# Turned rows of the hidden layer moved from an SBUF tile into PSUM, one step later, with quarter rows in two buffers

## The reference

```python
logits = x @ w_gate
e_idx = np.argmax(logits, axis=1)
...
for e in range(E):
    mask = e_idx == e
    h = np.maximum(x[mask] @ w1[e], 0.0)
    ye = h @ w2[e]
    out[mask] = gate_w[mask, None] * eom[mask, e, None] * ye
```

## Time and profile before

| what | value |
|---|---|
| median of 3 runs (lowest to highest) | 772.63 us (772.59 to 777.18) |
| the profiled execution's own time | 767.37 us |
| span of the profiled execution, first to last instruction | 765.7 us |
| TensorE busy | 719.5 us, 94% |
| VectorE busy | 492.6 us, 64% |
| ScalarE busy | 306.8 us, 40% |
| granted TensorE clock, mean | 0.99 of full speed |

### The profile page before, as it was taken

The page is one execution under the profiler, slowest core; times in us unless marked ns, Lnnn a source line. Parts: engine busy times, 40 slices in busy tenths (PEclk is TensorE's granted clock), DMA queues, the critical chain, the costliest instruction groups (busy, mean ns, idle before and its releaser), DMA issues.

```text
span 765.7 us, 16189 instructions
## 1 busy us (share of the span) xinstructions
PE 719.5 (94%) x5272; PEld 617.3 (81%) x5273; DVE 492.6 (64%) x777; ACT 306.8 (40%) x467; POOL 188.6 (25%) x352
## 2 busy tenths in 40 slices
PE   3899999999999999999988979999898989999995
PEld 3689998999899899989887767788686868788873
DVE  5787877787767676768716746536757575665441
ACT  3644443444344434443334434134444535363220
POOL 3211543345111211211211212122131312222111
PEclk9999999999999999999999999999999999999998
DMA  8723235323322231231017648442848485843230
GB/s 323 247 70 99 97 112 158 117 96 114 120 69 69 91 115 69 69 107 46 22 38 246 217 131 220 146 110 60 272 110 277 118 251 144 255 90 79 71 72 36
DMA packets 43949, 98.70 MB, mean 129 GB/s; under 512 B 6286, under 2 KB 19982, under 8 KB 43792
## 3 DMA queue, kind: packets, MB, share of 16 engines
q1 hardware_dynamic: 22128, 64.82, 26.2%
q10 hardware_dynamic: 15840, 16.52, 9.4%
q0 software_dynamic: 5952, 16.98, 7.5%
HBM read 73.78 MB, written 14.09 MB: 115 GB/s over the span
## 4 chain that ended last, share of the span: by engine, by line
PE 78%; DMA 7%; DVE 5%; issue 5%; ACTq 2%; DVEq 1%; ACT 1%; POOLq 0%; SPq 0%; POOL 0%
PE banks L1216 65%; DMA r_quads<-r_sb 5%; PE banks L1247 4%; PE banks L1237 3%; PE banks L1269 3%; PE banks L1229 2%; ACTq L724 2%; DVE slots_hi_lo L1162 1%; PE banks L1349 1%; DMA q_sb<-q_t 1%; ACT r_sb L717 1%; DVEq L406 1%; DMA xs<-x_rows,rows_now 1%; DVE xsT_lo L1044 0%; DVE ys_even L1170 0%
## 5 line engine op out<-in xcount | busy, mean ns | idle before, releaser
L1216 PE MATMUL banks<-slots_hi_lo,rT_hi 128*128 128x512 f32 x464 | 146.2, 396 | 2.9 <-DVE rT_lo L1055 2.2
L1216 PE MATMUL banks<-slots_hi_lo,xsT_hi 128*128 128x512 f32 x464 | 128.4, 399 | 15.5 <-DVE xsT_lo L1044 10.4
L1216 PEld LDWEIGHTS banks<-slots_hi_lo,xsT_hi 128*128 128x128 f32 x464 | 86.9, 191 | 39.3 <-issue 21.7
L1216 PEld LDWEIGHTS banks<-slots_hi_lo,rT_hi 128*128 128x128 f32 x464 | 84.8, 188 | 20.4 <-issue 3.1
L1216 PE MATMUL banks<-slots_hi_lo,rT_lo 128*128 128x512 f32 x232 | 90.6, 391 | 0.0
L1044 DVE TENSOR_TENSOR xsT_lo<-banks,xsT_hi 128x512 fp32r<-128x512 f32 x30 | 20.7, 690 | 102.5 <-ACT xsT_hi L695 102.5
L1216 PE MATMUL banks<-wout_hi,uT_hi 128*128 128x264 f32 x384 | 83.2, 298 | 2.0 <-DVE uT_lo L880 2.0
L1216 PE MATMUL banks<-wout_hi,uT_lo 128*128 128x264 f32 x384 | 78.6, 286 | 0.0
L1216 PE MATMUL banks<-wout_lo,uT_hi 128*128 128x264 f32 x384 | 78.4, 286 | 0.0
L1050 DVE STREAM_TRANSPOSE r_turned<-r_quads 128x1024 f32<-128x1024 f32 x26 | 52.5, 2021 | 35.0 <-DMA r_quads<-r_sb 34.0
L1216 PE MATMUL banks<-slots_hi_lo,xsT_lo 128*128 128x512 f32 x232 | 72.8, 396 | 0.0
(11 more groups left out here) (169 smaller groups left out, 1190.7 us busy)
## 6 DMA issues: line engine op xcount, KB each, us to landing
raw_w<-experts SPq DMA_DIRECT2D x56, 512.0 KB, 4.6
r_quads<-r_sb ACTq DMA_DIRECT2D x104, 128.0 KB
v_sb<-v_win SPq DMA_DIRECT2D x24, 384.0 KB, 4.8
k_sb<-k_win SPq DMA_DIRECT2D x22, 384.0 KB, 3.7
x_rows<-x SPq DMA_DIRECT2D x24, 264.0 KB, 2.1
q_sb<-q_t SPq DMA_DIRECT2D x24, 256.0 KB, 2.7
stage<-experts POOLq DMA_DIRECT2D x8, 512.0 KB, 6.3
weights<-w_both ACTq DMA_DIRECT2D x4, 512.0 KB, 10.3
```

The lines of the kernel that those rows point to most:

```text
L1216: ins = mm(o, lhs, rhs(part, k, n), start=(k == first and lhs is not None and part == 0 and parts == (0, 1)), stop=(k == final and parts = ...
```

## The change

`r_quads` becomes two buffers, used in turn by tile parity. The SBUF tile `r_turned` goes away; the turned rows are written to PSUM banks 2 and 3 (`turn_ps`), and `high_r` and `low_r` read them there. VectorE turns tile t-1 in step t, in front of low_r(t-1); the turn of the last tile moves to `ending`. On ScalarE the row copy xt(t+1) goes ahead of the four transfers of tile t, which now wait for the turn of tile t-2, and high_r(t-1) goes behind gate_exp(t+1). TensorE, GpSimd and SyncE are not touched.

```diff
@@ -233,8 +233,7 @@
         r_sb = rc.take("r_sb", [P, DF], F32)
         rT_hi += [rc.take("rT_hi1", [P, DF], F32R)]
         rT_lo += [rc.take("rT_lo1", [P, DF], F32R)]
-        r_quads = rc.take("r_quads", [P, DF], F32)
-        r_turned = rc.take("r_turned", [P, DF], F32)
+        r_quads = [rc.take(f"r_quads{n}", [P, DF], F32) for n in range(2)]
         ys = [rc.take("ys_even", [P, DM], F32), ys_odd]
         assert rc.at <= stage_at
 
@@ -719,9 +718,9 @@
             def quads_r(t):
 
                 act.wait_ge(relu_s, t.i + 1)
-                at_least(act, r_turn_s, t.i - BY_PE)
+                at_least(act, r_turn_s, t.i - (BY_PE + 1))
                 for a in range(QUADS):
-                    act.dma_start(r_quads[a * 32:(a + 1) * 32, :],
+                    act.dma_start(r_quads[t.par][a * 32:(a + 1) * 32, :],
                                   r_sb[:, a * (DF // QUADS):(a + 1) * (DF // QUADS)]).then_inc(r_quads_s, 16)
 
             def high_r(t):
@@ -732,7 +731,7 @@
                     nc.scalar.activation(rT_hi[t.par][:, :], turn_ps, ACT.Copy).then_inc(rthi_s, 1)
                 else:
                     act.wait_ge(r_turn_s, t.i - (BY_PE - 1))
-                    nc.scalar.activation(rT_hi[t.par][:, :], r_turned[:, :], ACT.Copy).then_inc(rthi_s, 1)
+                    nc.scalar.activation(rT_hi[t.par][:, :], turn_ps, ACT.Copy).then_inc(rthi_s, 1)
 
             def load_k(b):
                 act.dma_start(k_sb[b][:, :, :, :].rearrange("p a c n -> p (a c n)"), k_in[b, :, :]).then_inc(load_s[b], 16)
@@ -803,14 +802,14 @@
             def step_c(t):
                 found = next_experts(act, t)
                 relu(t)
-                if not by_pe(t):
-                    quads_r(t)
                 xt(t + 1)
                 if by_pe(t):
                     high_r(t)
-                elif not by_pe(t + -1):
+                else:
+                    quads_r(t)
+                gate_exp(t + 1)
+                if not by_pe(t) and not by_pe(t + -1):
                     high_r(t + -1)
-                gate_exp(t + 1)
                 if isinstance(t.i, int) and t.i == 2:
                     pieces(1, 1)
                 split_next(act, pieces, t, found)
@@ -1047,13 +1046,12 @@
 
                 dve.wait_ge(r_quads_s, (t.i - (BY_PE - 1)) * QUADS * 16)
                 dve.wait_ge(rtlo_s, t.i)
-                nc.vector.transpose(r_turned[:, :].rearrange("p (c j b) -> p b c j", c=KF, b=QUADS),
-                                    r_quads[:, :].rearrange("p (b c i) -> p b c i", b=QUADS, c=KF)).then_inc(r_turn_s, 1)
+                nc.vector.transpose(turn_ps.rearrange("p (c j b) -> p b c j", c=KF, b=QUADS),
+                                    r_quads[t.par][:, :].rearrange("p (b c i) -> p b c i", b=QUADS, c=KF)).then_inc(r_turn_s, 1)
 
             def low_r(t):
                 dve.wait_ge(rthi_s, t.i + 1)
-                nc.vector.tensor_tensor(rT_lo[t.par][:, :], turn_ps if by_pe(t) else r_turned[:, :],
-                                        rT_hi[t.par][:, :].bitcast(F32), ALU.subtract).then_inc(rtlo_s, 1)
+                nc.vector.tensor_tensor(rT_lo[t.par][:, :], turn_ps, rT_hi[t.par][:, :].bitcast(F32), ALU.subtract).then_inc(rtlo_s, 1)
 
             dve.wait_ge(mask_in_s, 16)
             softmax_a(At(0, 0))
@@ -1184,11 +1182,9 @@
                     low_r(t)
                     result(t + -1)
                     gate_value(t + 1)
-                elif by_pe(t + -1):
-                    turn_r(t)
-                else:
+                elif not by_pe(t + -1):
+                    turn_r(t + -1)
                     low_r(t + -1)
-                    turn_r(t)
                     result(t + -2)
                     gate_value(t)
                 if isinstance(t.i, int) and t.i == 2:
@@ -1196,6 +1192,7 @@
                 split_next(dve, pieces, t, found)
 
             def ending(t):
+                turn_r(t)
                 low_r(t)
                 result(t + -1)
                 result(t)
```

## The result

The changed kernel took 749.98 us (median of 4 runs, 747.71 to 751.12) beside 772.61 us for the kernel before (4 runs, 767.72 to 777.18); the ratio is 0.9704, 95% interval 0.964 to 0.9768. Two later groups of runs gave 0.9714 (0.9655 to 0.9773) and 0.9741 (0.9696 to 0.9785). The direction was as forecast, and so in the main was the mechanism; the size was not: 757.0 us was forecast and 752 was the lower bound.

What follows compares the result with a forecast made beforehand. TensorE was taken as the bound in undisturbed steps, 11.0 of 11.4 us, so only its pauses could be won. 1.9 + 2.0 + 10.1 + 3.4 - 1.8 = 15.6 us gave 757.0 us; own range 752 to 762, wider range 752 to 766.

Steps and rivals of the forecast that it cites:

- the same gain from the median: Whole kernel: the 15.6 us gained on the profiled 767.4 us, taken instead from the median of 772.63, gives 757.0 us.
- the turn one step later: Steps with weight splits: VectorE no longer waits for a landing, so all five pauses go; gain 10.1 us.
- the end: Behind the loop: the last tile's turn moves there and TensorE's last product starts later; loss 1.8 us.
- named pauses: Five TensorE pauses ahead of `hidden`, behind pairs of steps with weight splits, 10.1 us together, all forecast to go.
- Copy first: Steps 3 and 4: row copy ahead of the four transfers; gain 1.9 us and 2.0 of 2.99 us.
- The landing rival: Pair steps: relu(t+1) waits for tile t's transfers instead, about 1.5 us back at five pairs, 764.5 us; chance 0.11.
- The turn's price: VectorE's turn writing PSUM: taken as 2.0 us, as at present, between bounds of 1.2 and 4.0 us.
- the walk: Step-by-step timing of a pair of steps with weight splits, from its first input product; 2.7 us of slack remain.
- The doubling: Rival on VectorE: with a PSUM operand the turn takes 4.0 us, 9.8 us back, 766.8 us; chance 0.09.
- The clock: Two input products at halved TensorE clock, behind pauses that go: both stretches taken as gone, gain 3.4 us.

Runs made afterwards that it cites:

- padded kernel: The changed kernel with half of the turn's columns turned once beforehand, 0.72 + 1.26 us, against the changed kernel: 749.17 us beside 748.77 us.
- third profile: The third of three profiled executions of the changed kernel, with nothing changed in it; its steps 3 and 4 together took 20.4 us.

## Why the prediction fell short, step by step

The measured 749.98 us lies 7.0 us under the forecast, and two steps of the prediction carry that. The larger is the last one, "the same gain from the median": 4.7 us. The other is the term of 10.1 us for the turn one step later, which was 14.5 us; taken with the errors of the other terms, the sum was 2.3 us short.

| place | forecast, us | measured in the profiles, us |
|---|---|---|
| step 3, with its halved clock | -3.6 | -3.8 |
| step 4 | -2.0 | +1.1 |
| the 23 steps behind, with one halved stretch | -11.8 | -16.2 |
| the end | +1.8 | +1.0 |
| sum | -15.6 | -17.9 |

**Turn one step later: right, and mis-sized.** This is the term of the sum that failed. I took the gain as the 10.1 us of named pauses; the 23 steps lost 16.2 us, of which 1.7 us is the halved clock behind the first pair. So 14.5 us stand against 10.1. The view counts a pause from the modelled end of one matmul to the start of the next. In front of four of the five pauses the step before was also 0.3 to 0.4 us too long (11.65, 11.76, 11.67 and 11.69 us against 11.36), with no pause over 0.15 us named in it. A step with a pause of 1.73 us was 2.4 us too long (13.76 us); in it and in step 18 TensorE also stopped ahead of `expert_out`, by 0.4 and 0.9 us, of which the view names 0.62 us, and I had left that out. Step lengths from one recurring instruction would have given the right term.

**Copy first: right in step 3, wrong in step 4.** Step 3: 3.8 us measured against 1.9 + 1.7. In step 4 I expected a pause of 1.0 us and got 2.45. The place was right: ScalarE's relu waited 6.04 us for tile 3's transfers.

```profile
447.01 1.02 ACT L716 ACTIVATE r_sb<-banks 128x1024 f32<-128x1024 f32 x1 [6.04 <-DMA r_quads<-r_sb]
447.93 0.59 ACT L694 ACTIVATE xsT_hi<-banks 128x512 fp32r<-128x512 f32 x1
448.07 2.53 ACTq L723 DMA_DIRECT2D r_quads<-r_sb  x4
```

But from issue at 436.61 they took 10.4 us, not the 8.7 us of before. They vary, and so does the clock behind the pause: the padded kernel's step 4 took 9.15 us, with no named pause over 1 us, and the changed kernel's own 11.05 to 14.07 us. I had also taken the copy's place as worth something only in these two steps; it is worth about 11 us in all once relu can be late (760.25 against about 749).

**The landing rival** came true as a wait and not as a cost. ScalarE's relu waited for transfers five times, 28.6 us in all:

```profile
ACT r_sb L716 <- DMA r_quads<-r_sb: 28.6, 5, 6.0
```

The output product covered four of the five. What was forecast as 9.5 us from first issue to landing took 8.4 to 10.7 us beside weight loads and 5.3 to 6.2 us otherwise.

**The turn's price.** I took 2.0 us between bounds of 1.2 and 4.0; it was 1.25 us, near the lower bound. The padded turn shows that this hardly entered the time. There is luck in that: the wait for the high parts behind the turn, 1.1 to 1.5 us in the forecast, was 2.2 us on average (58.0 us over 26), as they also stand behind the issues and `gate_exp` on ScalarE. So turn and wait together, 3.5 us, came out as in the walk.

The doubling that I drew from the Trainium skill (VectorE: DVE Perf Modes, "Why PSUM operands drop a tier") did not show on a turn that writes PSUM. By the Trainium skill (Vector Engine (DVE) Microarchitecture Reference, section 3.8, one element per cycle and lane; VectorE: DVE Perf Modes, "Specifications", 0.96 GHz) 1024 columns are 1.07 us, an estimate. The trace comes near it, with 1.25 us into PSUM and 1.245 us straight into SBUF. What made it disagree before, with 2.02 us, was the stride of the write into SBUF.

**The clock.** I took 3.4 us for two halved stretches going. Both went, but two others came in this execution: behind the pause of step 4 and at the end, behind 1.92 us. Net nothing, and wrong to count in full while I forecast a pause of 1.0 us myself. It is chance as well, since the third profile has neither of the two.

**The end.** Loss of 1.8 us forecast, 1.0 us measured. The idle time in front of the code behind the loop stayed, with the turn now behind it:

```profile
724.53 1.23 DVE L1054 TENSOR_TENSOR rT_lo<-banks,rT_hi 128x1024 fp32r<-128x1024 f32 x1 [2.38 <-ACT rT_hi L734]
...
729.66 1.26 DVE L1049 STREAM_TRANSPOSE banks<-r_quads 128x1024 f32<-128x1024 f32 x1 [2.80 <-issue]
732.02 1.23 DVE L1054 TENSOR_TENSOR rT_lo<-banks,rT_hi 128x1024 fp32r<-128x1024 f32 x1 [1.09 <-ACT rT_hi L734]
```

2.80 us of it, as 2.70 us in the earlier trace rows. The pause of 1.7 us that I forecast ahead of the last product did not come. The product before it, part of it at halved clock, ran from 726.38 to 733.58 us, and the low parts were ready at 733.25. In the third profile, with no halved stretch there, a pause of 1.19 us came in its place and the end was as long, 29.3 us.

**The second buffer** I costed at nothing but as a means. Without it the same change is 2.4% slower than the kernel before. My walk had the high parts behind the issue, and so held the reason; I did not ask what that order would do with one buffer.

**From the profile to the median: the larger part of the miss.** In the profile the gain was 17.9 us against 15.6 forecast. The other 4.7 us of the difference come from the median that I subtracted from. The kernel before had its median 5.3 us above its profiled execution, the changed one only 0.5 us (749.98 and 749.5), and I carried the 5.3 us over whole. That median of 772.6 us was over few runs; 54 later ones of the same kernel had medians of 766.6 to 768.1 us. From 768 us the forecast would have been 752.4. In those later groups the gain by medians was 19.2 and 20.1 us, so the sum stays short there too. Why the first four runs were slower is open.

## What to carry to other kernels

Size a pause by the length of the step that it sits in, measured between starts of one recurring instruction, not by the idle time that the view names; and look at the step in front too. Do not carry a distance between one execution and a median of three over to the changed kernel. When a wait is moved off one engine, ask for each engine what now stands between the released work and its consumer: the issue of transfers (here 2.6 us for four) is work in an in-order list, and its place decided between 750 and 785 us. Parts that each give under 1% can give 2.6% to 3% together, so a part that fails alone is not refuted.

## What the runs showed of the hardware

- VectorE's 32 x 32 turn of 128x1024 fp32: 2.02 us when it writes every fourth column of an SBUF tile, 1.245 us when it writes the tile straight, 1.25 us when it writes every fourth column of two PSUM banks. Half of the columns into PSUM: 0.716 us.
- Four transfers of 128 KB issued by ScalarE hold its list for 2.5 to 3.0 us.
- In the changed kernel the last of the four landed 8.4 to 10.7 us after the first issue beside weight loads (11 times), 5.3 to 6.2 us otherwise (15 times).
- TensorE's clock went to half behind some of its pauses (1.93, 2.45, 2.53, 2.98 us) and not behind others (2.32, 2.76, 2.99 us). An input product with such a stretch took 7.20 us, one without 5.50 us.
- VectorE's first instruction behind the hardware loop began 2.7 us (before) and 2.8 us (after) after the last one in it.
